# A leaky activation in two ScalarE instructions per tile in place of three

## The chip, the cores and the metric

The kernel runs on one core of a Trainium2 chip. The metric is device time in microseconds (us). The engines are named as in the profile: PE is TensorE (PEld its weight loads), DVE is VectorE, ACT is ScalarE, POOL is GpSimd, SP is SyncE, which here issues DMAs. A change of under 0.3% can't be told from none.

## The reference

Three layers follow each other. The activation that the change touches is in the second.

```
scores = q @ k^T / 8                       # 4 batches x 8 heads, 576 x 576 each, head size 64
keep the 32 largest scores of each row; attn = softmax over them
x  = attn @ v, as 2304 rows of 512
h  = x @ w_in                              # 512 -> 2048
g  = max(h, 0) + alpha * min(h, 0)         # alpha: one number per column of h, drawn from 0 to 0.3
x2 = g @ w_out                             # 2048 -> 512
out = x2, and for the rows with x2 @ w_skip > 0, one of 8 experts (512 -> 1024 -> 512, ReLU)
      is added, weighted with its gate's probability
```

## The kernel before

**Attention.** Work goes in 16 passes of four heads and half the rows of a batch; a pass has nine tiles of 128 rows x 576 scores, in three groups of three tiles. PE makes the scores (L542, L547), ACT stores them (L835). DVE searches the 32nd largest score of each row: four rounds of MAX8 (L1050) with three of MATCH_REPLACE8 (L1063) between them. ACT takes the exponentials (L844) after the first round. DVE masks them and sums them, one SCALAR_TENSOR_TENSOR per tile (L1070, two inputs in SBUF). `invert` (L1079, L1082) makes one over the sums in two tiny DVE operations, put behind the first two MAX8 of the next group. POOL multiplies the tiles by that (L1324), PE transposes them (L560, L561), ACT stores those (L856, L857), and PE multiplies by v (L571).

**The MLP in between.** Two passes make one step of a loop, which runs over eight steps; step 0 has no MLP. From step 1 on, PE also computes the MLP of the half batch that is ready, in an order written out by hand: during the first pass of the step, sixteen tiles of `h` transposed (128 columns of h x 288 rows, twelve fp16 matmuls each, L590, because x and the weights are split into a high and a low fp16 part), during the second pass the product with w_out (L604), then the routing and the rows (L613, L619). There are eight halves: seven in the loop's steps, the eighth after the last attention pass, in the tail.

**The activation before.** For every tile ACT runs three instructions (L882, L883, L886):

```
pos_part = Relu(acc * scale)              # L882, from PSUM
neg_part = Relu(acc * -scale)             # L883, from PSUM, then acc_stored: PE may use the bank again
neg_part = neg_part * (-alpha)            # L886, in SBUF, after a wait for L883; then parts_ready
```

`leak` (L352) follows on POOL, or on DVE for the last half. It waits for parts_ready, adds the two parts (L358, two inputs in SBUF), rounds to fp16 (L360) and subtracts for the low part (L362). POOL does tiles 0 to 4 behind L1324 of the first group of a step, 5 to 11 behind the second, 12 to 15 behind the third (`leak_parts`, L1371). There are four buffers for the parts, and ACT waits for `g_ready` before it writes one again. The instruction order of each engine is fixed; an engine stops at semaphores only.

**Scales.** At the start DVE and ACT take maxima of the weights and of v, POOL spreads them to all partitions over DRAM, and DVE makes powers of two from them (`close_weights` L1097, `scale_weights` L1120). `link_scale` makes an operation of this chain raise a semaphore and DVE wait for it. In step 0 `high_weights` (L927) on ACT multiplies each of eight weight pieces of 128 x 2048 by its scale (L932) and writes the high fp16 part (L936); POOL's `split` (L1334, L1339) writes the low part. The pieces are spread over the groups of step 0, two to a group; the last four are w_out.

Of the kernel before, what the change touches and what calls it, by code (L numbers as in the profile page):

```python
# [24 lines left out]
def topk_attention_prelu_mlp_switch_moe(  # L25
# [17 lines left out]
    ALU = mybir.AluOpType  # L43
    ACT = mybir.ActivationFunctionType
# [53 lines left out]
    with ctx:  # L98
        def sb(name, shape, dt=fp32):
            return ctx.enter_context(nc.sbuf_tensor(name, shape, dt))  # L100
# [69 lines left out]
        neg_scale_g = sb("neg_scale_g", [P, 1])  # L170
        x2_scale = sb("x2_scale", [P, 1])
        neg_alpha = sb("neg_alpha", [P, FT1])
# [111 lines left out]
        parts_ready = sem("parts_ready")  # L284
# [67 lines left out]
        def leak(engine, unit, m, fs):  # L352

            for f in fs:
                n = LEAK_STEPS * (FT1 * m + f)
                pos, neg = pos_part[:, f % NEG, :], neg_part[:, f % NEG, :]
                hold(engine, parts_ready, FT1 * m + f + 1)
# [454 lines left out]
        def _(act):  # L812
# [63 lines left out]
            def mlp_part(m, items, par, part):  # L876
                if par == 0:
                    for f in range(FT1 * part // PARTS, FT1 * (part + 1) // PARTS):
                        n = FT1 * m + f
                        src = begin(items)  # L880
                        act.wait_ge(g_ready, n + 1)
                        nc.scalar.activation(pos_part[:, f % NEG, :], src[:, 0:HALF], ACT.Relu, scale=scale[:, 3:4])  # L882
                        nc.scalar.activation(neg_part[:, f % NEG, :], src[:, 0:HALF], ACT.Relu, scale=neg_scale_g[:, 0:1])\  # L883
                            .then_inc(acc_stored, 1)
                        act.wait_ge(acc_stored, items.base + items.used)
                        nc.scalar.activation(neg_part[:, f % NEG, :], neg_part[:, f % NEG, :], ACT.Copy, scale=neg_alpha[:, f:f + 1])\  # L886
                            .then_inc(parts_ready, 1)
# [39 lines left out]
            def high_weights(i, par, g, half):  # L927
                for n in split_slots.get(GROUPS * (2 * i + par) + g, ())[half:half + 1] if isinstance(i, int) and i < MLP_LAG else ():
                    k = 1 if n < DT else 2
                    act.wait_ge(scale_ready, 1)  # L930
                    act.wait_ge(raw_loaded[n], 16)
                    nc.scalar.activation(raw[:, n, :], raw[:, n, :], ACT.Copy, scale=scale[:, k:k + 1]).then_inc(w_scaled, 1)  # L932
# [101 lines left out]
        def _(dve):  # L1034
# [62 lines left out]
            def close_weights():  # L1097
# [4 lines left out]
                nc.vector.tensor_scalar(neg_alpha[:, :], alpha_sb[:, :], -1.0, None, ALU.mult)  # L1102
# [17 lines left out]
            def scale_weights():  # L1120
                dve.wait_ge(spread_loaded, 16)
                scale_of(1, 3).then_inc(scale_ready, 1)
# [5 lines left out]
                nc.vector.tensor_scalar(neg_scale_g[:, :], scale[:, 3:4], -1.0, None, ALU.mult)  # L1128
# [33 lines left out]
            for m in range(HALVES - MLP_LAG, HALVES):  # L1162
                leak(dve, nc.vector, m, range(FT1))
# [139 lines left out]
        def _(pool):  # L1303
# [68 lines left out]
            with pool.Fori(MLP_LAG, STEPS) as i:  # L1372
                for par in range(2):
                    for g in range(GROUPS):
# [3 lines left out]
                        leak(pool, nc.gpsimd, i - MLP_LAG, leak_parts.get((par, g), ()))  # L1378
# [76 lines left out]
```

## Time and profile before

| what | us |
|---|---|
| median of three runs | 1118.12 |
| lowest and highest | 1116.74, 1120.65 |
| the profiled execution | 1123.2 |
| its span | 1121.4 |
| PE busy | 927.9 (83%) |
| DVE busy | 903.8 (81%) |
| ACT busy | 631.4 (56%) |
| POOL busy | 427.4 (38%) |

The shares are averages over stages of different kinds. Up to about 150 us the weights are made ready beside the first two passes. From 150 to 876 us DVE searches and the MLP runs beside it. From 897 to 950 the last half of the MLP runs alone, and then the experts take the rest of the span. What an engine's busy time is worth has to be read in the stage where it lies.

### The profile page before, as it was taken

The page shows a single profiled execution, that of the slowest core. Times are in us where ns is not written, and L with a number is a line of the kernel's source. Part 1 is how long each engine was busy: PE and PEld are TensorE (multiplying, and loading weights), DVE is VectorE, ACT ScalarE, POOL GpSimd, SP SyncE. Part 2 cuts the span into 40 slices and gives each one's busy share as a digit, 9 for nine tenths or more (in the row PEclk, how much of TensorE's full clock was granted, in tenths as well). Part 3 has the DMA queues.
Part 4 walks back from the last instruction along what each step waited for, and adds up shares of the span by engine and source line. Part 5 has one row for each costly group of instructions (what it writes and reads, how often), then busy time and mean ns, then how long its engine had stood idle before and what let it go on. Part 6 is the DMA issues. An engine that isn't in the chain of part 4 may idle for free.

```text
span 1121.4 us, 22533 instructions
## 1 busy us (share of the span) xinstructions
PE 927.9 (83%) x6271; PEld 616.9 (55%) x6272; DVE 903.8 (81%) x1984; ACT 631.4 (56%) x1324; POOL 427.4 (38%) x598
## 2 busy tenths in 40 slices
PE   5346588898899889888988898899888889498996
PEld 2223256675666657665766575667556567243342
DVE  4999989999999999999999999999999270611110
ACT  3786969647855785587459637954883281010100
POOL 0136738514830682267028513840582100201110
PEclk9956589999999999999999999999999799699999
DMA  7910110013002200310031004001100166626650
GB/s 205 365 37 22 32 34 22 23 41 87 0 21 70 57 0 21 96 32 21 1 97 30 21 8 119 1 21 53 44 2 1 55 226 213 221 90 225 199 165 18
DMA packets 98658, 84.05 MB, mean 75 GB/s; under 512 B 69116, under 2 KB 77308, under 8 KB 98048
## 3 DMA queue, kind: packets, MB, share of 16 engines
q1 hardware_dynamic: 94544, 78.56, 23.0%
q0 software_dynamic: 1488, 3.15, 0.8%
q10 hardware_dynamic: 2528, 1.18, 0.4%
q8 instruction: 43, 0.70, 0.3%
q14 instruction: 55, 0.45, 0.1%
HBM read 72.64 MB, written 11.53 MB: 75 GB/s over the span
## 4 chain that ended last, share of the span: by engine, by line
PE 62%; POOL 12%; issue 11%; ACT 8%; DVE 4%; DMA 2%; POOLq 1%; ACTq 0%; DVEq 0%
PE acc L604 16%; PE acc L571 8%; PE sc L542 7%; PE pt_full L560 6%; PE acc L590 5%; POOL pos_part L358 5%; PE sc L712 3%; PE pt_full L772 3%; POOL arena L360 3%; POOL arena L1324 2%; PE pt_full L780 2%; PE sc L721 2%; PE acc L613 2%; ACT arena L844 1%; PE acc L619 1%
## 5 line engine op out<-in xcount | busy, mean ns | idle before, releaser
L1050 DVE MAX8 best<-arena 128x8 f32<-128x576 f32 x576 | 403.5, 742 | 9.8 <-ACT arena L835 6.6
L1063 DVE MATCH_REPLACE8 arena<-best,arena 128x576 f32<-128x576 f32 x432 | 315.8, 738 | 0.0
L1324 POOL TENSOR_SCALAR arena<-arena,row_inv 128x576 f32<-128x576 f32 x144 | 106.5, 757 | 351.3 <-DVE row_inv L1082 351.3
L590 PE MATMUL acc<-arena 128*128 (+1 forms) x1536 | 202.4, 286 | 28.0 <-ACT neg_part L883 26.1
L604 PE MATMUL acc<-arena 128*128 128x288 f16 x1536 | 202.2, 289 | 2.9 <-issue 2.9
L590 PEld LDWEIGHTS acc<-arena 128*128 128x128 f16 x1536 | 146.4, 98 | 78.8 <-issue 38.9
L604 PEld LDWEIGHTS acc<-arena 128*128 128x128 f16 x1536 | 149.6, 99 | 49.6 <-issue 12.9
L560 PE MATMUL pt_full<-ident,arena 128*128 128x128 f32 x576 | 102.4, 306 | 60.0 <-POOL arena L1324 34.4
L835 ACT ACTIVATE arena<-sc 128x576 f32<-128x576 f32 x144 | 92.1, 642 | 87.1 <-PE sc L542 70.6
L1070 DVE SCALAR_TENSOR_TENSOR arena<-arena,best 128x576 f32<-128x576 f32 x144 | 126.7, 927 | 5.9 <-ACT arena L844 5.9
L560 PEld LDWEIGHTS pt_full<-ident,arena 128*128 128x128 f32 x576 | 73.1, 155 | 90.3 <-POOL arena L1324 42.9
L542 PE MATMUL sc<-kT,qT 64*128 64x288 f32 x512 | 113.0, 478 | 7.0 <-ACT arena L835 5.0
L358 POOL TENSOR_TENSOR pos_part<-pos_part,neg_part 128x288 f32<-128x288 f32 x112 | 96.6, 863 | 48.6 <-ACT neg_part L886 48.6
L571 PE MATMUL acc<-arena,nat 128*64 128x288 f32 (+1 forms) x640 | 92.9, 431 | 20.4 <-ACT arena L857 13.7
L844 ACT ACTIVATE arena<-arena,neg_max 128x576 f32<-128x576 f32 x144 | 101.2, 765 | 1.6
L856 ACT ACTIVATE arena<-pt_full 128x512 f32<-128x512 f32 x128 | 75.5, 590 | 44.3 <-PE pt_rest L561 42.3
L362 POOL TENSOR_TENSOR arena<-pos_part,arena 128x288 f16<-128x288 f32 x112 | 86.7, 774 | 16.7 <-POOL arena L360 1.1
L542 PEld LDWEIGHTS sc<-kT,qT 64*128 64x128 f32 x512 | 63.1, 210 | 39.3 <-issue 20.1
L571 PEld LDWEIGHTS acc<-arena,nat 128*64 128x64 f32 (+1 forms) x640 | 45.0, 141 | 65.0 <-issue 49.8
L882 ACT ACTIVATE pos_part<-acc,scale 128x288 f32<-128x288 f32 x128 | 63.4, 495 | 26.6 <-PE acc L590 25.8
L886 ACT ACTIVATE neg_part<-neg_part,neg_alpha 128x288 f32<-128x288 f32 x128 | 68.5, 535 | 4.2
L883 ACT ACTIVATE neg_part<-acc,neg_scale_g 128x288 f32<-128x288 f32 x128 | 63.1, 493 | 0.0
(172 smaller groups left out, 942.2 us busy)
## 6 DMA issues: line engine op xcount, KB each, us to landing
arena<-in_moe_w_dram SPq DMA_DIRECT2D x64, 512.0 KB, 4.2
nat<-in_v_dram SPq DMA_DIRECT2D x64, 128.0 KB, 2.2
nat<-in_k_dram SPq DMA_DIRECT2D x60, 128.0 KB, 2.8
x_rows<-x2n SPq DMA_DIRECT2D x24, 192.0 KB, 2.4
out_dram<-x2n SPq DMA_DIRECT2D x24, 192.0 KB, 2.6
nat<-in_q_dram SPq DMA_DIRECT2D x64, 64.0 KB, 2.1
arena<-in_moe_w_in_dram SPq DMA_DIRECT2D x4, 1024.0 KB, 7.4
arena<-in_moe_w_out_dram SPq DMA_DIRECT2D x4, 1024.0 KB, 14.5
```

The source lines that it names most:

```text
L358: unit.tensor_tensor(pos, pos, neg, ALU.add).then_inc(leak_ready, 1)
L542: last = nc.tensor.matmul(dst[:, c, 0:HALF], qT[at, h // 2, r * P:(r + 1) * P], kT[at, h // 2, c * HALF:(c + 1) * HALF], start=True, stop= ...
L560: nc.tensor.transpose(pt_full[:, kt, :], src[:, kt * P:(kt + 1) * P], ident[:, :])
L571: last = nc.tensor.matmul(dst[h * D:(h + 1) * D, 0:HALF], v_nat[0:rows, par, 2 * c + h, kt, :], probsT[0:rows, 2 * c + h, kt, :], start=(k ...
L590: last = nc.tensor.matmul(dst[:, 0:HALF], win16[:, a, d, f * P:(f + 1) * P], xT16[:, bass.ds(row + d, 1), b, :].rearrange("p b s -> p (b s)"),
L604: last = nc.tensor.matmul(items.open[:, 0:HALF], wout16[:, a, f // (FT1 // OUT_CHUNKS), f % (FT1 // OUT_CHUNKS) * DM + d * P:f % (FT1 // O ...
L835: nc.scalar.activation(scores[:, t, :].rearrange("p (c s) -> p c s", c=2), sc[(TILES * par + t) % 2][:, :, 0:HALF], ACT.Copy).then_inc(s_s ...
L844: nc.scalar.activation(probs[:, gp, j, :], scores[:, GROUP * g + j, :], ACT.Exp, bias=neg_max[:, gp, j:j + 1], scale=SCALE).then_inc(exp_r ...
L1050: nc.vector.max(best[:, gp, j, r, :], src).then_inc(max_found if r == 0 else dve_step, 1)
L1063: nc.vector.match_replace(left[:, j, :], best[:, gp, j, r, :], src, MASKED).then_inc(dve_step, 1)
L1070: nc.vector.scalar_tensor_tensor(out=probs[:, gp, j, :], in0=tiles[j], scalar=best[:, gp, j, ROUNDS - 1, 7:8], in1=probs[:, gp, j, :], op0 ...
L1324: nc.gpsimd.tensor_scalar(probs[:, gp, j, :], probs[:, gp, j, :], row_inv[:, gp, j:j + 1], 1.0, ALU.mult, ALU.mult)\
```

## The change

With slope = alpha and bend = 1 - alpha, `alpha * h + Relu((1 - alpha) * h)` is h for positive h and alpha * h for negative h. ACT now makes `pos_part` as slope times h (a Copy with a column as scale) and `neg_part` as Relu of bend times h, both from PSUM, and the third instruction goes. For an alpha over 1 a sign is needed, which goes into slope and into the rows of w_out: so w_out's pieces are scaled by a column per 128 rows, in four instructions of 128 x 512 in place of one of 128 x 2048. DVE makes slope, bend and sign at the start. The semaphore parts_ready goes; `leak` waits for acc_stored, which counts tiles of all kinds, so its caller gives the number of the first.

```diff
-                hold(engine, parts_ready, FT1 * m + f + 1)
+                hold(engine, acc_stored, first_item + f + 1)
                 unit.tensor_tensor(pos, pos, neg, ALU.add).then_inc(leak_ready, 1)
...
-                        nc.scalar.activation(pos_part[:, f % NEG, :], src[:, 0:HALF], ACT.Relu, scale=scale[:, 3:4])
-                        nc.scalar.activation(neg_part[:, f % NEG, :], src[:, 0:HALF], ACT.Relu, scale=neg_scale_g[:, 0:1])\
+                        nc.scalar.activation(pos_part[:, f % NEG, :], src[:, 0:HALF], ACT.Copy, scale=slope[:, f:f + 1])
+                        nc.scalar.activation(neg_part[:, f % NEG, :], src[:, 0:HALF], ACT.Relu, scale=bend[:, f:f + 1])\
                             .then_inc(acc_stored, 1)
-                        act.wait_ge(acc_stored, items.base + items.used)
-                        nc.scalar.activation(neg_part[:, f % NEG, :], neg_part[:, f % NEG, :], ACT.Copy, scale=neg_alpha[:, f:f + 1])\
-                            .then_inc(parts_ready, 1)
...
-                    nc.scalar.activation(raw[:, n, :], raw[:, n, :], ACT.Copy, scale=scale[:, k:k + 1]).then_inc(w_scaled, 1)
+                    if n < DT:
+                        last = nc.scalar.activation(raw[:, n, :], raw[:, n, :], ACT.Copy, scale=scale[:, 1:2])
+                    else:
+                        for f in range((n - DT) * FT1 // OUT_CHUNKS, (n - DT + 1) * FT1 // OUT_CHUNKS):
+                            at = slice(f % (FT1 // OUT_CHUNKS) * DM, (f % (FT1 // OUT_CHUNKS) + 1) * DM)
+                            last = nc.scalar.activation(raw[:, n, at], raw[:, n, at], ACT.Copy, scale=sign[:, f:f + 1])
+                    last.then_inc(w_scaled, 1)
...
-                nc.vector.tensor_scalar(neg_alpha[:, :], alpha_sb[:, :], -1.0, None, ALU.mult)
+                link_scale(nc.vector.tensor_scalar(slope[:, :], alpha_sb[:, :], 1.0, None, ALU.min))
+                link_scale(nc.vector.tensor_scalar(sign[:, :], alpha_sb[:, :], 1.0, -2.0, ALU.is_gt, ALU.mult))
+                link_scale(nc.vector.tensor_scalar(sign[:, :], sign[:, :], 1.0, None, ALU.add))
+                link_scale(nc.vector.tensor_tensor(slope[:, :], slope[:, :], sign[:, :], ALU.mult))
+                link_scale(nc.vector.tensor_scalar(bend[:, :], alpha_sb[:, :], -1.0, 1.0, ALU.mult, ALU.add))
...
-                scale_of(1, 3).then_inc(scale_ready, 1)
+                link_scale(scale_of(1, 3))
+                nc.vector.tensor_scalar(sign[:, :], sign[:, :], scale[:, 2:3], None, ALU.mult).then_inc(scale_ready, 1)
...
-                nc.vector.tensor_scalar(neg_scale_g[:, :], scale[:, 3:4], -1.0, None, ALU.mult)
+                nc.vector.tensor_scalar(slope[:, :], slope[:, :], scale[:, 3:4], None, ALU.mult)
+                nc.vector.tensor_scalar(bend[:, :], bend[:, :], scale[:, 3:4], None, ALU.mult)
```

## Rows read from the trace of the kernel before

**Rows 1.** The chain that ended last, its shares of the span by engine.
```profile
PE 62%; POOL 12%; issue 11%; ACT 8%; DVE 4%; DMA 2%; POOLq 1%; ACTq 0%; DVEq 0%
```
**Rows 2.** Windows, DVE alone: window, length, DVE busy (count), clock, DMA share, GB/s.
```profile
255.40:361.20 105.80, 104.41 (x230) 0.98 0.15 40
...
678.70:784.30 105.60, 104.08 (x229) 0.98 0.15 39
```
**Rows 3.** Groups by line: line engine op out<-in xcount | busy us, mean ns | idle before.
```profile
L844 ACT ACTIVATE arena<-arena,neg_max 128x576 f32<-128x576 f32 x144 | 101.2, 765 | 1.6
...
L886 ACT ACTIVATE neg_part<-neg_part,neg_alpha 128x288 f32<-128x288 f32 x128 | 68.5, 535 | 4.2
L882 ACT ACTIVATE pos_part<-acc,scale 128x288 f32<-128x288 f32 x128 | 63.4, 495 | 26.6 <-PE acc L590 25.8 <-POOL arena L362 0.5
...
L871 ACT ACTIVATE x<-acc,scale 128x288 f32<-128x288 f32 x32 | 16.1, 502 | 42.3 <-PE acc L571 42.3
```
**Rows 4.** Timeline of DVE: start us, us, instruction, [idle before it <- releaser].
```profile
184.78 1.16 DVE L1070 SCALAR_TENSOR_TENSOR arena<-arena,best 128x576 f32<-128x576 f32 x1 [0.32 <-ACT arena L844]
...
714.25 1.16 DVE L1070 SCALAR_TENSOR_TENSOR arena<-arena,best 128x576 f32<-128x576 f32 x1 [0.33 <-ACT arena L844]
```
**Rows 5.** Timeline of ACT in the third step of the loop.
```profile
377.45 2.11 ACT L844 ACTIVATE arena<-arena,neg_max 128x576 f32<-128x576 f32 x3
...
380.48 0.49 ACT L883 ACTIVATE neg_part<-acc,neg_scale_g 128x288 f32<-128x288 f32 x1
381.00 0.54 ACT L886 ACTIVATE neg_part<-neg_part,neg_alpha 128x288 f32<-128x288 f32 x1
```
**Rows 6.** Timeline of POOL in the same step.
```profile
381.68 0.81 POOL L358 TENSOR_TENSOR pos_part<-pos_part,neg_part 128x288 f32<-128x288 f32 x1 [1.94 <-ACT neg_part L886]
...
397.29 1.31 POOL L358 TENSOR_TENSOR pos_part<-pos_part,neg_part 128x288 f32<-128x288 f32 x1
...
400.66 0.79 POOL L358 TENSOR_TENSOR pos_part<-pos_part,neg_part 128x288 f32<-128x288 f32 x1
```
**Rows 7.** Two lines of DVE, each by itself: durations in ns, min/median/max.
```profile
L1070 DVE SCALAR_TENSOR_TENSOR arena<-arena,best x144: 790/812/1432, 31.6 to 874.8; 128x576 f32<-128x576 f32 x144
...
L1079 DVE TENSOR_SCALAR row_den<-row_sum x48: 141/150/773, 41.0 to 875.6; 128x3 f32<-128x3 f32 x48
```
**Rows 8.** Timeline of DVE in the same step as rows 5 and 6.
```profile
379.28 1.07 DVE L1070 SCALAR_TENSOR_TENSOR arena<-arena,best 128x576 f32<-128x576 f32 x1
...
396.78 1.16 DVE L1070 SCALAR_TENSOR_TENSOR arena<-arena,best 128x576 f32<-128x576 f32 x1 [0.34 <-ACT arena L844]
...
397.88 1.33 DVE L1070 SCALAR_TENSOR_TENSOR arena<-arena,best 128x576 f32<-128x576 f32 x1
...
399.14 0.96 DVE L1070 SCALAR_TENSOR_TENSOR arena<-arena,best 128x576 f32<-128x576 f32 x1
...
400.71 0.77 DVE L1079 TENSOR_SCALAR row_den<-row_sum 128x3 f32<-128x3 f32 x1
...
419.18 0.59 DVE L1079 TENSOR_SCALAR row_den<-row_sum 128x3 f32<-128x3 f32 x1
```
**Rows 9.** Timeline of DVE before the first step with an MLP.
```profile
48.89 0.16 DVE L1102 TENSOR_SCALAR neg_alpha<-alpha_sb 128x16 f32<-128x16 f32 x1
...
58.66 0.15 DVE L1125 TENSOR_SCALAR power<-spread 128x1 int32<-128x1 int32 x1
58.85 0.15 DVE L1126 TENSOR_SCALAR scale<-power 128x1 int32<-128x1 int32 x1
...
150.46 0.82 DVE L1070 SCALAR_TENSOR_TENSOR arena<-arena,best 128x576 f32<-128x576 f32 x1 [3.37 <-ACT arena L844]
```
**Rows 10.** Timeline of ACT: the scaling of a piece of w_out.
```profile
119.90 1.99 ACT L932 ACTIVATE arena<-arena,scale 128x2048 f32<-128x2048 f32 x1
```
**Rows 11.** Timeline in the tail: the last tile's add, and w_out's first matmuls.
```profile
921.87 0.46 DVE L358 TENSOR_TENSOR pos_part<-pos_part,neg_part 128x288 f32<-128x288 f32 x1 [0.17 <-ACT neg_part L886]
...
923.27 11.90 PE L604 MATMUL acc<-arena 128*128 128x288 f16 x83 [2.93 <-issue]
```

More of the change, by code:

```diff
@@ L169, in topk_attention_prelu_mlp_switch_moe @@
         unscale = sb("unscale", [P, 4])
-        neg_scale_g = sb("neg_scale_g", [P, 1])
         x2_scale = sb("x2_scale", [P, 1])
-        neg_alpha = sb("neg_alpha", [P, FT1])
+        slope = sb("slope", [P, FT1])
+        bend = sb("bend", [P, FT1])
+        sign = sb("sign", [P, FT1])
         x32 = sb("x32", [P, 2, HALF])
@@ L283, in topk_attention_prelu_mlp_switch_moe @@
         x2_written = sem("x2_written")
-        parts_ready = sem("parts_ready")
         leak_ready = sem("leak_ready")
@@ L350, in topk_attention_prelu_mlp_switch_moe, with leak @@
         LEAK_STEPS = 2
-        def leak(engine, unit, m, fs):
+        def leak(engine, unit, m, first_item, fs):
             for f in fs:
@@ L928, in high_weights @@
                 for n in split_slots.get(GROUPS * (2 * i + par) + g, ())[half:half + 1] if isinstance(i, int) and i < MLP_LAG else ():
-                    k = 1 if n < DT else 2
                     act.wait_ge(scale_ready, 1)
                     act.wait_ge(raw_loaded[n], 16)
-                    nc.scalar.activation(raw[:, n, :], raw[:, n, :], ACT.Copy, scale=scale[:, k:k + 1]).then_inc(w_scaled, 1)
+                    if n < DT:
[5 more added lines that the diff above has]
+                    last.then_inc(w_scaled, 1)
                     act.wait_ge(w_scaled, n + 1)
@@ L1162, in _ @@
             for m in range(HALVES - MLP_LAG, HALVES):
-                leak(dve, nc.vector, m, range(FT1))
+                leak(dve, nc.vector, m, TAIL_BASE + PV_ITEMS, range(FT1))
             def link(ins):
@@ L1377, in _ @@
                             low_x(2 * i + par - 1)
-                        leak(pool, nc.gpsimd, i - MLP_LAG, leak_parts.get((par, g), ()))
+                        leak(pool, nc.gpsimd, i - MLP_LAG, LOOP_BASE + (i - MLP_LAG) * FULL_ITEMS + PV_ITEMS + PREP_ITEMS, leak_parts.get((par, g), ()))
             low_x(PASSES_A - 1)
```

## The prediction

> **What bounds the kernel now.** I read the chain of waits first [rows 1]. It gives 62% of the span to PE and 12% to POOL, with ACT at 8%. In a loop where two engines hand work back and forth, such a chain can run along either, so I set the busy times of one loop pass beside it [rows 2]. DVE is busy for 104.4 of 105.8 us in the first and for 104.1 of 105.6 in the last of the five passes from 255 to 784 us. DVE is the bound of the loop: ACT may lose work there without moving the end. So the three ACT instructions of a tile are not priced by their sum. What counts is (a) where DVE waits for ACT, (b) what DVE's own instructions cost, (c) the start, where ACT, POOL and PE form the chain and DVE waits, and (d) the tail, where DVE has little to do.
>
> **The instruction removed.** L886 ran 128 times at 535 ns, 68.5 us of ACT [rows 3]. The Relu L882 becomes a Copy with a column as scale; L871 is such a Copy from PSUM of the same 128x288 and takes 502 ns against 495. That edit costs nothing. Almost all of the 68.5 us lies beside DVE's search and is worth zero.
>
> *(a) DVE's waits for ACT in the loop.* L844 (the exponentials) is queued on ACT behind the tile work. DVE stands 0.32 to 0.34 us for it before one L1070, once in each of six passes (the first and the last of them in [rows 4]). ACT reaches L844 earlier by at least one L886 (0.53 us), so this wait goes: 6 x 0.33 = 2.0 us. After it DVE has only its own work.
>
> *(b) DVE's own instructions.* L1070 takes 0.81 us at its median but up to 1.43, and L1079, a tiny operation, takes 0.15 at its median and up to 0.77 [rows 7]. The slow ones stand beside POOL's leak operations. In one pass: L1070 at 396.78, 397.88 and 399.14 takes 1.16, 1.33 and 0.96, that is 0.35 + 0.52 + 0.15 = 1.0 us more than three medians [rows 8]; POOL's L358, started at 397.29, takes 1.31 instead of its usual 0.80 [rows 6]. L1079 at 400.71 takes 0.77, and POOL's L358 occupies 400.66 to 401.45: L1079 ends when that ends, 0.62 lost. At 419.18 another L1079 takes 0.59 (0.44 lost). The first L1070 at 379.28 loses 0.26. With the three L1070 at the head of the second half (about 1.0 again) that is some 3.4 us in a pass. The pattern is that of taking turns: whichever engine came second stands until the other's instruction is through. What the change does here depends on phase alone, and it shifts POOL's phase.
>
> The shift: the third tile's L883 starts on ACT at 380.48, its L886 at 381.00 and ends at 381.54, and POOL's add starts at 381.68 [rows 5, 6]. After the change POOL waits for the second instruction only (0.53 earlier), and ACT, which had worked without a gap since the tile before, has done one L886 less (0.53 again, and a little of the overlap). POOL's add starts near 380.56, 1.1 us earlier. Now by turns:
> - First window (L1070 from 379.28): the add of tile 1 no longer touches it, gain 0.26. The add at 380.56 now comes in front of the third L1070, which loses 0.52 as the one at 397.88 did, and POOL's subtraction L362, about 2 us after the add with POOL's own stalls in between, then meets L1079 (0.45). Net +0.7.
> - POOL's later tiles run back to back behind this one, so they move earlier by 1.1 less what POOL lost in that window (0.4): 0.7. Second window: DVE starts it 0.7 later but without the 0.33 wait. It now falls so that the first L1070 waits for nothing, the second for 0.15, the third for 0.5: 0.65 in place of 1.0, and L1079 falls at the end of an add (0.05 in place of 0.62). Net -0.33 -0.35 -0.57, and DVE stands 0.6 ahead of before.
> - Third window (L1070 near 415): both engines are 0.6 to 0.7 earlier, same phase, same losses, 0.
>
> Sum of a pass: 0.7 - 0.33 - 0.35 - 0.57 = -0.55, with some -0.6 by the finer addition; over six passes with the wait -3.6 and the seventh without it -0.3: **-3.9 us** for (a) and (b) together. The bounds: if the first window costs 0.7 and nothing is given back, a pass is +0.36 and the loop +2.5; if both hits on L1079 vanish (1.06) with some 0.5 of the L1070s' loss, a pass is -1.1 with half the wait's gain left in it and the loop -8. I take the value that follows the rows at 380.48 and 381.68, since the phase up to there is set by PE, and repeats in every pass.
>
> The Trainium skill (SBUF — State Buffer, section on the two separate sides) says that DVE and GpSimd share one port pair, as an exclusive lock held for a whole instruction, for a DVE operation with two SBUF inputs among others. By that rule the phase decides, as I reckoned above; by a port whose bandwidth is divided, only the overlap would count, and the loop would give about -1.5. L1079, which ends with POOL's add though it moves three numbers, speaks for the lock.
>
> **The edits at the start, all costs.** *DVE.* In place of one unlinked operation (L1102, after which the next starts 0.08 later) come five linked ones. Linked ones of this size follow each other at 0.19 (58.66 to 58.85) [rows 9]: 5 x 0.19 - 0.08 = +0.87. In the scale step one operation gets a link (+0.12), sign times scale comes (+0.07), and two multiplications replace one (+0.07): +0.26. Together +1.1 on DVE at 49 to 59 us. The maxima go to POOL and back by DMA, and DVE's and POOL's next steps all start from these, so the whole chain moves by it.
> *ACT.* Each of the four pieces of w_out is scaled by four instructions of 512 columns instead of one of 2048, which takes 1.99 [rows 10]. From this 2048 and the 288 of L886 (535 ns), both with a column as scale: (1990-535)/1760 = 0.83 ns per column, so 512 columns take 0.72; consecutive ones overlap by 0.1 (L844: three in 2.11 where one takes 0.765 [rows 3, 5]), so 3 x 0.62 + 0.72 = 2.58, +0.6 a piece. Lower bound: no fixed part, +0; upper: no overlap, 2.88, +0.9. Three of the four pieces have ACT on the chain behind them, one has a PE wait of 0.57 that hides it: +1.8. DVE will not hide it: DVE waits at 150.46 for 3.37 us, for ACT's L844 [rows 9], so the chain over ACT, POOL and PE ends last there, and DVE's wait becomes some 5.2. The start costs 1.1 + 1.8 = **+2.9 us**, bounds +1.1 and +3.8.
>
> **The tail.** In the last half's sixteen tiles PE runs from tile to tile without a stop and does not get faster. Only the end moves: DVE's add of the last tile starts at 921.87, just behind L886, and PE starts L604 at 923.27 after standing 2.93 [rows 11]. With L886 gone this is 0.53 earlier: **-0.5 us**. It would be 0 if PE's instruction stream were what stands there, 1.1 if ACT had run one tile behind.
>
> **Sum.** +2.9 - 3.9 - 0.5 = -1.5. The profiled execution took 1123.2 (its span 1121.4 and 1.8 around it) and would take 1121.7. The median of the runs is 1118.1, 5.1 lower with nothing in the trace to say which stage; I carry the difference over: 1116.7.
>
> **Rivals.**
> - *DVE is the bound and POOL's phase brings little* (shared bandwidth, or the hits only move about). For it: the windows are crowded anyway. Against: L1079 at 0.77. Loop -1.5, start +2.9, tail -0.5: +0.9, 1119.0. Chance 0.17.
> - *Relief is larger*: in the first window L1079 misses the subtraction by 0.15 us, which is 0.45 less in each of seven passes: -1.5 - 3.1 = -4.6, 1113.5. A shift in the phase of 0.15 us decides it. Chance 0.22.
> - *Slower*: POOL's earlier adds fall on DVE's L1070 in the first window (+0.7 a pass) and nothing is given back in the second. It decides as soon as the 0.33 and the relief of the second window together fall under 0.3. Loop +2.5, start +2.9, tail -0.5: +4.9, 1123.0. Against it: POOL's whole later stream moves with DVE's. Chance 0.15.
> - *ACT was the bound and gives its time back*, 68.5 us less 2.4: 1052. Against it, DVE busy for 104.4 of 105.8. Chance 0.01. That the edit doesn't shorten ACT's queue at all (Copy at a higher price than Relu) has no row for it and is within the first rival.
>
> **How the numbers follow.** The forecast's case has 0.45, and its own range is 1114 to 1119. A measurement here tells 0.3% (3.35 us) from no change, so faster is under 1114.8 and slower over 1121.5. Faster: all of the larger relief and a sixth of the forecast's case, 0.30. Slower: most of the fourth case and the edges of two others, 0.16. Same: 0.54. The range of eight in ten reaches from the larger relief to just short of the slower case's centre: 1111 to 1122.
>
> **What would show it.** L886 gone, L882 at 0.49 to 0.50. DVE's wait near 150 grown to about 5. POOL's third add 1.1 us earlier against DVE's L1070, the third L1070 of that window at 1.33; no wait of 0.33 before the next window; the sum of L1079's time lower. A pass of about 105.3. The gap before the last half's L604 at 2.4. I am wrong if a pass stays at 105.8 or grows, or if the start costs nothing because DVE's wait there doesn't grow.

## The result, and the profile after

| us | before | after |
|---|---|---|
| median (runs) | 1118.28 (6) | 1126.99 (6) |
| lowest and highest | 1116.64, 1120.65 | 1123.24, 1131.82 |
| the profiled execution, its span | 1123.2, 1121.4 | 1131.8, 1130.0 |
| ACT, DVE, PE busy | 631.4, 903.8, 927.9 | 571.5, 904.8, 939.8 |

The ratio is 1.008, interval [1.0051, 1.0109]: slower by 8.7 us where 1.5 us faster was forecast, and outside the range of 1111 to 1122. The two profiled executions stand 8.6 apart, so they can stand for the runs. ACT did lose 60 us of work. (Ratios leave out runs of more than 1.5% above their kernel's fastest, five of twelve in e11 and three of twelve in e3; these may be part of the effect, so both ratios can understate it.)

The groups by line of the changed kernel (columns as in [rows 3]); ACT's queue is as expected:
```profile
L1072 DVE SCALAR_TENSOR_TENSOR arena<-arena,best 128x576 f32<-128x576 f32 x144 | 130.0, 950 | 16.8 <-ACT arena L844 16.6
...
L882 ACT ACTIVATE pos_part<-acc,slope 128x288 f32<-128x288 f32 x128 | 63.9, 499 | 78.0 <-PE acc L590 61.2
L844 ACT ACTIVATE arena<-arena,neg_max 128x576 f32<-128x576 f32 x144 | 101.2, 765 | 1.6
...
L883 ACT ACTIVATE neg_part<-acc,bend 128x288 f32<-128x288 f32 x128 | 63.2, 494 | 0.0
```
L1072 is the old L1070. DVE stood 16.6 us for L844 ahead of it. Where, the windows of DVE show, one for each of five steps of the loop (a step, two attention passes, is what the prediction calls a pass; columns as in [rows 2]):
```profile
257.30:362.30 105.00, 103.72 (x229) 0.97 0.15 40
362.30:471.30 109.00, 104.70 (x229) 0.94 0.15 38
471.30:578.00 106.70, 104.24 (x230) 0.98 0.15 39
578.00:683.10 105.10, 104.06 (x230) 0.97 0.15 39
683.10:792.20 109.10, 104.78 (x230) 0.94 0.14 37
```
Two steps are shorter than any before (105.6 to 106.0 in windows cut alike), as forecast; three are 1 to 3 us longer, and in them DVE isn't busier to match but stands. DVE's timeline in the second and third of these steps shows for what:
```profile
366.55 0.82 DVE L1072 SCALAR_TENSOR_TENSOR arena<-arena,best 128x576 f32<-128x576 f32 x1 [2.23 <-ACT arena L844]
420.05 0.82 DVE L1072 SCALAR_TENSOR_TENSOR arena<-arena,best 128x576 f32<-128x576 f32 x1 [0.68 <-ACT arena L844]
...
474.80 0.82 DVE L1072 SCALAR_TENSOR_TENSOR arena<-arena,best 128x576 f32<-128x576 f32 x1 [1.42 <-ACT arena L844]
```
ACT, though it has less to do, is late: it waits for PE. The windows of PE (the column after the count is the granted clock), cut where the clock falls and rises, first the kernel before:
```profile
353.10:356.50 3.40, 3.40 (x15) 0.50 0.54 169
```
and the changed one, in the heads of four steps:
```profile
249.40:252.80 3.40, 3.40 (x15) 0.50 0.54 167
355.20:368.90 13.70, 12.52 (x47) 0.50 0.56 151
464.50:471.30 6.80, 6.80 (x24) 0.50 0.72 213
570.30:573.70 3.40, 3.40 (x15) 0.50 0.46 143
```
In every step PE falls to 1.2 GHz (0.50) once, just after the routing product L613, 24 matmuls of nine columns. In the kernel before it is back at 2.4 GHz after 3.4 us, in all six steps. In the changed kernel it stays at 1.2 GHz for 3.4, 13.7, 6.8, 3.4, 13.6 and 13.7 us. What lies there takes longer: forty L571 took 5.52 at 361.24 before, and, with the first 3.5 us of them inside the slow stretch, 7.22 after:
```profile
365.40 7.22 PE L571 MATMUL acc<-arena,nat 128*64 128x288 f32 x40 [1.18 <-ACT arena L857]
```
The sum over DVE's timeline: from the first masking after the start (150.46 before, 153.25 after) to the head of the step at 771.31 (779.51), 620.85 us became 626.26, +5.4; the start +2.8; from there to PE's first L604 of the tail (923.27, 932.29) +0.8; all behind that -0.4. Together 8.6. The +0.8 hides two things: DVE's own last step, with a wait of 2.58 in it, grew by 3.6 (its last masking ends at 875.57 and 887.32), and PE made up 2.7 of it. Of the +5.4, three undisturbed steps gave -0.4 to -0.6 each, and the three disturbed ones took +3.2, +0.5 and +3.1.

### The profile page after: what moved, and what is told of

It is laid out like the page before. It is cut to its first block, busy times and chain, and to the rows that moved or that the text cites. A ratio compares the mean times of both kernels' runs of the same rounds, so it can differ in the third digit from the quotient of the medians.

```text
span 1130.0 us, 22423 instructions
## 1 busy us (share of the span) xinstructions
PE 939.8 (83%) x6271; PEld 621.7 (55%) x6272; DVE 904.8 (80%) x1990; ACT 571.5 (51%) x1208; POOL 432.9 (38%) x598
## 4 chain that ended last, share of the span: by engine, by line
PE 55%; POOL 12%; issue 11%; ACT 10%; DMA 7%; DVE 2%; SPq 1%; POOLq 1%; ACTq 0%; DVEq 0%
PE acc L604 16%; PE acc L571 8%; PE sc L542 7%; DMA arena<-in_moe_w_dram 5%; POOL pos_part L358 5%; PE pt_full L560 5%; PE acc L590 4%; POOL arena L360 3%; PE sc L712 2%; POOL arena L1332 2%; PE pt_full L772 2%; PE acc L613 2%; POOL arena L1347 1%; ACT arena L844 1%; DMA arena<-in_moe_w_out_dram 1%
## 5 line engine op out<-in xcount | busy, mean ns | idle before, releaser
L604 PE MATMUL acc<-arena 128*128 128x288 f16 x1536 | 202.6, 289 | 2.4 <-issue 2.4
L604 PEld LDWEIGHTS acc<-arena 128*128 128x128 f16 x1536 | 149.7, 99 | 49.2 <-issue 12.3
L1072 DVE SCALAR_TENSOR_TENSOR arena<-arena,best 128x576 f32<-128x576 f32 x144 | 130.0, 950 | 16.8 <-ACT arena L844 16.6
L542 PE MATMUL sc<-kT,qT 64*128 64x288 f32 x512 | 118.5, 499 | 6.4 <-ACT arena L835 4.8
L571 PE MATMUL acc<-arena,nat 128*64 128x288 f32 (+1 forms) x640 | 98.4, 451 | 20.8 <-ACT arena L857 13.9
L882 ACT ACTIVATE pos_part<-acc,slope 128x288 f32<-128x288 f32 x128 | 63.9, 499 | 78.0 <-PE acc L590 61.2
L844 ACT ACTIVATE arena<-arena,neg_max 128x576 f32<-128x576 f32 x144 | 101.2, 765 | 1.6
L362 POOL TENSOR_TENSOR arena<-pos_part,arena 128x288 f16<-128x288 f32 x112 | 88.4, 789 | 16.6 <-POOL arena L360 1.1
L571 PEld LDWEIGHTS acc<-arena,nat 128*64 128x64 f32 (+1 forms) x640 | 46.9, 147 | 69.2 <-issue 55.2
L883 ACT ACTIVATE neg_part<-acc,bend 128x288 f32<-128x288 f32 x128 | 63.2, 494 | 0.0
L360 POOL TENSOR_SCALAR arena<-pos_part 128x288 f16<-128x288 f32 x112 | 55.1, 492 | 19.0 <-POOL pos_part L358 19.0
## 6 DMA issues: line engine op xcount, KB each, us to landing
arena<-in_moe_w_out_dram SPq DMA_DIRECT2D x4, 1024.0 KB, 13.6
```

The lines of the kernel that those rows point to most:

```text
L542: last = nc.tensor.matmul(dst[:, c, 0:HALF], qT[at, h // 2, r * P:(r + 1) * P], kT[at, h // 2, c * HALF:(c + 1) * HALF], start=True, stop= ...
L571: last = nc.tensor.matmul(dst[h * D:(h + 1) * D, 0:HALF], v_nat[0:rows, par, 2 * c + h, kt, :], probsT[0:rows, 2 * c + h, kt, :], start=(k ...
L604: last = nc.tensor.matmul(items.open[:, 0:HALF], wout16[:, a, f // (FT1 // OUT_CHUNKS), f % (FT1 // OUT_CHUNKS) * DM + d * P:f % (FT1 // O ...
L844: nc.scalar.activation(probs[:, gp, j, :], scores[:, GROUP * g + j, :], ACT.Exp, bias=neg_max[:, gp, j:j + 1], scale=SCALE).then_inc(exp_r ...
L1072: nc.vector.scalar_tensor_tensor(out=probs[:, gp, j, :], in0=tiles[j], scalar=best[:, gp, j, ROUNDS - 1, 7:8], in1=probs[:, gp, j, :], op0 ...
```

## The experiments

All were timed in five rounds beside the kernel before, whose medians in these sessions were 1118.7 to 1120.6; ratios are to it. "Wait" is DVE's, for L844. After the profile my theory was: **the loop lost because PE stays slow at some heads, and DVE has no slack against the chain over PE and ACT there.** Rivals: the start alone; the DVE/POOL port; the new order on ACT.

**1. exps early.** In steps with an MLP part, the exponentials of the next pass's first group go ahead of that group's stores, in the changed kernel and in the kernel before.
```diff
-                            if j == 0 and not mlp:
+                            if j == 0:
                                 exps(p, par, 0)
...
-                        if mlp:
-                            exps(p, par, 0)
```


> The changed kernel with one move on ACT: in steps with an MLP the exponentials of a pass's first group are issued ahead of the stores of the last group's tiles of the pass before, as in step 0, and no longer behind them. Theory 'clock': what is lost in the loop is that PE stays at 1.2 GHz for up to 13.6 us at the head of some steps, that ACT's exponentials stand in its queue behind stores that wait for this PE, and that DVE waits for them (2.2 to 2.6 us in three steps, 5.1 at the first). Then the waits of DVE for the exponentials at the heads of steps vanish even where PE stays slow: 5.1 at the start, 6.2 to 9 in the loop; about 1127 - 10 = 1117, between 1113 and 1119, faster than the kernel before or level with it. Theory 'port' (DVE's masking is slower by POOL's earlier adds, 130.0 against 126.7 us busy): only the wait at the first step goes, about 1122. Theory 'start only': same, 1122.

> The kernel before with the same move of the exponentials as the first of these runs. It takes away DVE's wait of 3.4 us at 150 us and nothing in its later steps, where DVE didn't wait at the head. All theories: about 1118.3 - 3.4 = 1115. If its steps stay 105.8 long, theory 'clock' expects no long slow stretch to matter; if they come, DVE doesn't wait for them.

Measured 1144.5, 1.021 [1.018, 1.024], and 1160.0, 1.036 [1.033, 1.039]. Both wrong. The waits at the head went, and greater ones came one group later, in both; the kernel before now had one in each step (its timeline of DVE; the masking line is L1069 here):
```profile
391.19 0.82 DVE L1069 SCALAR_TENSOR_TENSOR arena<-arena,best 128x576 f32<-128x576 f32 x1 [5.18 <-ACT arena L844]
```
The three exponentials, 2.1 us of ACT [rows 5], put ahead of the stores delay PE's whole chain. So that chain has no room to spare in the old kernel either; "DVE is the bound" was half of the truth. The steps of e4 took 112.1 to 113.2 us. That is more than the 2.1 that were moved, and PE was at 1.2 GHz for only 3.4 us in those of 112.1 to 112.4; where the rest comes from isn't shown.

**2. The same by one store only**: exps goes just ahead of the last store of scores.

> The changed kernel; in the steps with the second layer, exps of the next pass's first group is issued ahead of the last store of scores of the previous group, and not behind it: it comes about 0.5 us earlier on ScalarE, and only that one store (whose scores VectorE wants last) comes 2.3 us later. If what VectorE lacks at the head of a step after a long stretch of TensorE at 1.2 GHz is only that exps came late, each such wait (1.2 to 2.6 us) gets 0.5 shorter and the kernel gives some 1125 (2 us less). The rival, by the two kernels with exps at the head of the group (1144 and 1160): the chain over ScalarE and TensorE has no room for a shift, the last store is late for the next search, and the time stays at 1127 or grows, with waits for L844 or for the stored scores in the middle of the step.

> The kernel before with the same shift of exps by one store. If room is there, its six waits of 0.33 for L844 shrink or stay and the time is 1117 to 1119. By the rival (the chain is level with VectorE) new waits come in the middle of the step and the time grows past 1122.

Measured 1129.0, 1.0086 [1.0066, 1.0107], and 1121.0, 1.0011 [0.9999, 1.0024]. Nothing gained; in e17 the waits after a slow stretch were 3.3 in place of 2.2 to 2.6, the step still 109.0 to 109.3, and the rival held. e18 fell between its two figures (1119 and 1122) and has no new wait for L844 in the loop, only five of 0.31 to 0.32.

**3. Which part of the change?** e3 scales w_out's pieces by one instruction again, e11 takes the whole start from the kernel before (both leave the sign of an alpha over 1 out, and no alpha is over 0.3), and e12 gives the kernel before the four short instructions only.
```diff
-                        for f in range((n - DT) * FT1 // OUT_CHUNKS, (n - DT + 1) * FT1 // OUT_CHUNKS):
-                            at = slice(f % (FT1 // OUT_CHUNKS) * DM, (f % (FT1 // OUT_CHUNKS) + 1) * DM)
-                            last = nc.scalar.activation(raw[:, n, at], raw[:, n, at], ACT.Copy, scale=sign[:, f:f + 1])
+                    k = 1 if n < DT else 2
+                    nc.scalar.activation(raw[:, n, :], raw[:, n, :], ACT.Copy, scale=scale[:, k:k + 1]).then_inc(w_scaled, 1)
```


> The changed kernel, but each piece of w_out is scaled by one ACT instruction of 2048 columns as before; it leaves out the sign in w_out's rows, which is 1 everywhere for these slopes. By the prediction's step for the start, the wait of DVE at 153 us falls from 5.1 to about 3.3 and the first step with an MLP starts 1.8 us earlier. Theory 'start only': 1125. Theory 'clock, by phase': the first 1.8 us come off too, but the steps also end at other times, so the number of long slow stretches changes in an unforeseen way: between 1116 and 1129.

> The loop part of the change alone: two ACT instructions per tile as in the changed kernel, but at the start DVE makes slope and bend in as many linked steps as before, and each piece of w_out is scaled by one instruction; it leaves out the sign for slopes over 1. By the prediction's steps the start costs 0.1 instead of 2.9 us (DVE's wait near 150 us back to 3.4, the first masking after it at 150.5), and steps without a long stretch are 105.2. Theory 'clock, by phase': long stretches all the same, 1117 to 1130 with a wide spread, median about 1124. Theory 'start only' (the start's 2.8 us and what follows from it are the loss): 1115.

> A start part of the change alone: the kernel before with each piece of w_out scaled by four instructions. By the prediction's step, +1.8 us at the start: DVE's wait near 150 us grows from 3.4 to 5.2. Steps stay 105.8 long. Theory 'clock, by phase': as the slow stage of PE before 150 us carries the start's shift into the step ends, their place can change once, but steps of 105.8 keep it in all steps alike: all short (1120.5) or, if the new place is a bad one, nearly all long (1140). Rival: 1120.5.

Measured 1130.9, 1.0066 [1.0032, 1.0100]; 1132.7, 1.0052 [1.0017, 1.0086]; 1121.0, 1.0018 [0.9989, 1.0047]. e3 and e11 lie above what was expected of them. In e11 the start's cost is gone and the waits are there, at the same places as in the changed kernel:
```profile
148.91 0.82 DVE L1067 SCALAR_TENSOR_TENSOR arena<-arena,best 128x576 f32<-128x576 f32 x1 [3.31 <-ACT arena L844]
...
363.49 0.82 DVE L1067 SCALAR_TENSOR_TENSOR arena<-arena,best 128x576 f32<-128x576 f32 x1 [2.24 <-ACT arena L844]
416.99 0.82 DVE L1067 SCALAR_TENSOR_TENSOR arena<-arena,best 128x576 f32<-128x576 f32 x1 [0.68 <-ACT arena L844]
```
and in e12 only the start's cost:
```profile
152.85 0.82 DVE L1075 SCALAR_TENSOR_TENSOR arena<-arena,best 128x576 f32<-128x576 f32 x1 [4.94 <-ACT arena L844]
```
So the loop part alone brings most of the loss, and the start alone little. The size of the start's cost can't be read from single pairs such as 153.25 against 150.83 (e3) or 152.85 against 150.46: with one and the same start the first masking moves by 2.5 us between profiles (see 7).

**4. Is it the step's length, or ACT's order?** Dead MAX8 instructions on DVE change the length and leave ACT alone: at the end of the step (e2, 480 columns), behind the first pass's third group (e5, and e6 in the kernel before, 512), behind the second pass's second group (e9, e10 in the kernel before, 512; e16, 256).
```diff
+                        if par == 1 and g == 1:
+                            nc.vector.max(spare[:, :], left[:, 0, 0:512])
```


> The changed kernel with one dead instruction on DVE in each step of the loop: a MAX8 over 480 columns into a tile that nobody reads, about 0.56 us, which makes a step without a disturbance as long as before (105.8 instead of 105.2). Theory 'clock, by phase': whether PE's slow stretch at the end of a step is short (3.2 to 3.6 us) or long (6.8, 13.6) depends on when in time the step ends; with steps of 105.8 us all six of the kernel before were short. Then more work makes it faster: long stretches get rare, and the time is about 1118.3 + 2.8 (start) - 0.5 (tail) = 1120.5, 4 to 6 us under the changed kernel. Any theory in which the loop's loss comes from the shorter ACT queue itself, or from the port: 7 x 0.56 = 3.9 us more than the changed kernel, 1131.

> The changed kernel with one dead MAX8 on DVE (512 columns, 0.59 us) in each step of the loop, now inside the step, behind the search of the first pass's third group, where DVE runs without a gap: the dead instruction at the end of the step fell into the idle 1.1 us that DVE has there, and steps without a disturbance stayed at 105.2 to 105.3. Now they are 105.8 to 105.9, as in the kernel before. Theory 'clock, by phase' (short or long stretch at 1.2 GHz depends on when a step ends, and steps of 105.8 keep a good one good): fewer long stretches, faster than the changed kernel in spite of 4 us more work: 1118 to 1123, with a smaller spread. Rival 'the shorter ACT queue makes PE's pattern worse whatever the length of the step': 1127 + 4 = 1131.

> The kernel before with the same dead instruction: steps of 106.4. Work alone: 1119 + 7 x 0.59 = 1123. Theory 'clock, by phase': the good place in time is lost, long stretches come in some steps, 3.3 to 3.7 us each: 1126 to 1132, and a spread as wide as the changed kernel's. Rival: 1123, and every stretch stays at 3.2 to 3.6 us.

> The changed kernel with the dead MAX8 (512 columns, 0.61 us) behind the search of the second pass's second group, where POOL has no leak work that could give the time back by port, and where PE's work for the step's end starts from DVE. The dead instruction of the runs before lay beside POOL's work and was paid back there (L1079 took 0.18 us behind it instead of 0.77), so that steps stayed at 105.2 and 105.8. Now a step without a long stretch is 105.8 to 105.9. Theory 'clock, by phase': stretches at 1.2 GHz stay short where they begin short, median 1118 to 1124 and below the changed kernel's 1127, in spite of 7 x 0.6 us of added work. Rival (the shorter ACT queue itself makes long stretches likely, at any length of the step): 1127 + 4 = 1131, steps of 109.5.

> The kernel before with the same instruction at the same place: steps of 106.4 to 106.5. Work alone gives 1118.7 + 4.3 = 1123, stretches staying at 3.2 to 3.6 us (rival). Theory 'clock, by phase': long stretches in some steps, as in the changed kernel, 1126 to 1134, and a wider spread of the runs than the 7 us of the kernel before.

> The changed kernel with the dead MAX8 at the same place as in the ninth of these runs, of 256 columns (0.33 us): steps of 105.5 to 105.6 without a long stretch, between the changed kernel's 105.2 and the 106.2 of the ninth. Theory 'length of the step': fewer long stretches than the changed kernel or none, 2 to 6 us under it. Rival: 2.3 us over it.

| | median | ratio | undisturbed step | slow stretches at six heads |
|---|---|---|---|---|
| e2 | 1130.1 | 1.0078 [1.0053, 1.0102] | 105.2 | 3.4, 13.6, 13.6, 6.8, 3.4, 13.7 |
| e5 | 1129.5 | 1.0100 [1.0079, 1.0122] | 105.2 | 3.4, 13.7, 13.6, 13.7, 6.9, 3.5 |
| e6 | 1119.0 | 1.0011 [0.9992, 1.0031] | 105.8 | six of 3.4 |
| e9 | 1125.3 | 1.0042 [1.0013, 1.0071] | 106.1 | 3.4, 3.4, 3.5, three with no fall |
| e10 | 1128.3 | 1.0069 [1.0046, 1.0092] | 106.1 | three with no fall, three of 3.4 |
| e16 | 1129.6 | 1.0072 [1.0035, 1.0110] | 105.4 | 3.4, 3.4, 13.6, 13.7, 6.9, 3.5 |

In e2, e5 and e6 the dead work was hidden, in the idle time at the step's boundary or under the port, so the step kept its length and they tested nothing but that. In e9's profile the step is 106.1 to 106.3, and two ScalarE instructions give no long stretch and no wait at a head. The three heads with no fall have none because it moved: falls of 3.4 us lie inside the step, at 517.17 and 622.98, 105.8 apart. With 105.4 to 105.7 (e16) the long stretches come back. By the medians e9 (1125.3) lies just above its theory's range and under the rival's 1131, in spite of 4.3 us of added work: 1.0042 [1.0013, 1.0071] against 1.0103 [1.0071, 1.0135] for the changed kernel in 7. e16 missed: it was to gain 2 to 6 us by fewer long stretches, and has three of them and no gain clear of noise. e10 missed as well: it was to have long stretches and has none, yet it lost 7.7 us where 4.3 us of work were added.

**5. Shorten the old kernel's step.** One tiny DVE operation less in each `invert` (the 1e-9 left out), in the kernel before (e13) and the changed one (e14).
```diff
-                    nc.vector.tensor_scalar_add(row_den[:, gp, :], row_sum[:, gp, :], 1e-9).then_inc(den_ready, 1)
...
-                    nc.vector.reciprocal(row_inv[:, gp, :], row_den[:, gp, :]).then_inc(inv_ready, 1)
+                    nc.vector.reciprocal(row_inv[:, gp, :], row_sum[:, gp, :]).then_inc(inv_ready, 1)
```


> The kernel before, with its three ACT instructions per tile, but without L1079: DVE takes the reciprocal of the row sums directly (it leaves out the 1e-9 in the denominator). That instruction stood for POOL's adds twice in a step, for 0.62 and 0.44 us, and cost 0.06 four more times: steps get about 1.0 us shorter, 104.8. Theory 'length of the step': long stretches at 1.2 GHz now come in this kernel too, DVE waits for L844 at the heads of those steps (2.2 to 2.7 us, never seen in a kernel with three instructions), and the median is 1119 to 1130 in spite of 7 us less work. Rival 'the shorter ACT queue': no long stretches, 1119 - 8 = 1111.

> The changed kernel without L1079, in the same way (the 1e-9 is left out). Steps without a long stretch of about 104.7. Both theories leave long stretches possible: rival 1127 - 5 = 1122 with as many long stretches as the changed kernel; by 'length of the step' their number changes and can't be foretold, 1115 to 1130.

Measured 1119.4, 0.9998 [0.9975, 1.0021], and 1124.0, 1.0041 [1.0013, 1.0068]. e13 missed: the step is 105.7, not 104.8. DVE had 0.9 us less to do in a step, and stood instead (its timeline):
```profile
398.04 1.14 DVE L1070 SCALAR_TENSOR_TENSOR arena<-arena,best 128x576 f32<-128x576 f32 x1 [0.38 <-ACT arena L844]
416.53 0.82 DVE L1070 SCALAR_TENSOR_TENSOR arena<-arena,best 128x576 f32<-128x576 f32 x1 [0.63 <-ACT arena L844]
```
The chain over PE, ACT and POOL, with its fall of 3.4 us in it, is as long as DVE's work in this kernel: about 105.7 a step. e14 missed too: its steps are 105.3 to 106.1, not 104.7. Here the falls, 3.4 long and 105.8 apart, lie in the middle of the step (305.58, 411.40, ...), and DVE waits behind each, 2.0 us for four of five:
```profile
312.04 1.07 DVE L1072 SCALAR_TENSOR_TENSOR arena<-arena,best 128x576 f32<-128x576 f32 x1 [2.01 <-ACT arena L844]
```
So a short stretch, free at a head, costs a wait when it lies elsewhere. This profile is of one of the shorter executions (1117.5, where the median is 1124.0).

**6. Take the fall away.** Fourteen idle fp16 matmuls of 224 columns stand around L613.
```diff
+                fill(8)
...
+                    fill(3 if j else 0)
```


> The changed kernel, with eight idle fp16 matmuls of 224 columns on PE ahead of the routing product of each half (into unused columns of the bank; they lie in the 0.7 us in which PE waits for the last x2T), and three ahead of its second and third group of four matmuls: 0.6 us more on PE in the stage. The routing product is 24 matmuls of 9 columns, and the fall to 1.2 GHz follows on it in every step of both kernels. Theory 'clock': PE falls less often or not at all there, DVE's waits of 2.2 to 2.6 us at the heads of steps go, 1127 - 6 to - 9 = 1118 to 1121. If the fall isn't caused by this stage: 1127 to 1131.

> The kernel before with the same idle matmuls. Its stretches at the ends of steps were short (3.2 to 3.6 us) and DVE hardly waited for them, so little can be won: 1116 to 1120 by theory 'clock'. If the idle matmuls only cost, 7 x 0.6 us on a chain that is level with DVE: 1123.

Measured 1124.7, 1.0049 [1.0025, 1.0074], and 1122.1, 1.0024 [1.0001, 1.0046]. Most falls went, but each kernel has a long stretch at another place (13.7 us at 466.08 and 10.2 at 673.54), with a greater wait: 8.37, and 7.53 in the kernel before. So a kernel with three instructions can meet a long stretch too. Its steps without one are 105.5. DVE in the changed kernel:
```profile
477.42 0.82 DVE L1082 SCALAR_TENSOR_TENSOR arena<-arena,best 128x576 f32<-128x576 f32 x1 [8.37 <-ACT arena L854]
```
By this and e14 a slow stretch seems to cost DVE the more, the further it lies inside the step; no run moved one stretch on its own. The changed kernel's median is 2.3 us lower than without the idle matmuls, but the intervals overlap (1.0025 to 1.0074 and 1.0051 to 1.0109), and it stays behind the kernel before.

**7. The changed kernel once more.**

> The changed kernel itself, unaltered, as the mark for this chip: 1123 to 1132, three to four of six heads of steps with a long stretch.

Measured 1129.9, 1.0103 [1.0071, 1.0135]; stretches 3.4, 13.7, 13.6, 6.8, 3.4, 13.7, nearly the pattern of the first profile. The loop lost the same +5.4 in this profile: from the first masking at 151.08 to the head at 777.30, 626.22 us. The start's +2.8 did not repeat, it is +0.6:
```profile
151.08 0.82 DVE L1072 SCALAR_TENSOR_TENSOR arena<-arena,best 128x576 f32<-128x576 f32 x1 [4.77 <-ACT arena L844]
```
Over all profiles whose start and whose order on ACT are the changed kernel's (after, e2, e5, e7, e9, e14, e15, e16) this masking lies at 150.7 to 153.3, with 151.8 in the middle; over those with the old start (before, e6, e8, e10, e13) at 149.3 to 150.5, with 150.4 in the middle. The start costs some 1.4 us by these middles.

**What a profiled time holds besides.** All that follows from the start of the eighth L613, the routing and the experts, took 165.9 us (e9) to 173.7 (e16) in the twenty profiles, and not by kernel: 172.3 in the kernel before, 167.2 in e6, which has the same steps. The start of that L613 is the better mark of what the change does. The kernel before, the changed kernel and its second profile:
```profile
949.11 2.21 PE L613 MATMUL acc<-wroute,x2T 128*96 128x9 f32 x24 [0.59 <-ACT x2T L890]
958.11 2.21 PE L613 MATMUL acc<-wroute,x2T 128*96 128x9 f32 x24 [0.59 <-ACT x2T L887]
955.78 2.21 PE L613 MATMUL acc<-wroute,x2T 128*96 128x9 f32 x24 [0.59 <-ACT x2T L887]
```
It starts at 949.1 in e6, 949.4 in e14, 952.4 in e9, 954.2 in e10, 955.0 in e11, 955.7 in e16 and 962.6 in e3. The medians, less that of the kernel before in their session, follow roughly: +0.3, +4.3, +4.7, +7.7, +12.1, +9.8 and +11.6. e9's profiled execution took only 1120.0, the best but one of its twelve, because its experts took the least.

**What goes with 3.4 and what with 13.6.** Laid side by side, the sixteen profiles that have L613 in its usual surroundings (without e1, e4, e7, e8) show 84 falls at a head (e14 has its falls elsewhere in the step). What I read in each is the distance from the start of L613 to the fall, as in the first of these two rows of e16's PE and its windows:
```profile
350.34 0.82 PE L614 MATMUL acc<-wroute,x2T 128*96 128x9 f32 x8 [0.68 <-ACT x2T L888]
...
455.84 0.39 PE L614 MATMUL acc<-wroute,x2T 128*96 128x9 f32 x3 [0.68 <-ACT x2T L888]
```
```profile
353.30:356.70 3.40, 3.40 (x14) 0.50 0.57 176
459.10:472.70 13.60, 12.29 (x46) 0.50 0.57 152
```
The distance is 2.96 in the one, and 3.26 in the next. The fall is read to 0.1 us here and in the table; in finer windows 52 stretches of 3.4 us have distances of 1.84 to 2.99, and 32 stretches of 6.8 us and more have 3.09 to 3.58 (those of 6.8 the greatest, 3.50 and above). No case of these lies on the wrong side. It holds for the six heads inside the loop only: at the seventh, where the loop ends and other work follows, e3 has 2.75 and a stretch of 13.7. By step, with the step that follows:

| | distance, fall to fall | step |
|---|---|---|
| before | 2.97, 2.85, 2.80, 2.76, 2.74, 2.72; falls 105.8 apart | 105.6 to 106.1 |
| after | 2.86, 3.45, 3.56, 2.56, 3.24, 3.35; falls 105.8, 109.2, 105.8, 105.8, 109.2 apart | 105.35, 109.07, 106.63, 105.11, 109.08 |
| e13 | 2.14, 2.24, 2.34, 2.48, 2.58, 2.72 | 105.5 to 105.9 |
| e16 | 2.64, 2.96, 3.26, 3.48, 3.54, 2.58 | 105.44, 105.72, 108.72, 109.14, 106.80 |

The falls do not keep the kernel's time. They recur 105.8 us apart though the step is 105.3, so the distance grows by the difference, about 0.5 a step, until it passes 3.0 and PE stays slow. That step is long, the one after 6.8 us throws the distance back by 1.0, and it starts again. The kernel before has a step of 105.8, the same as the distance between falls: its L613 keeps its place, at a good one. Whether that is an accident isn't shown. e6, e12, e13 and e18 have 105.7 to 105.8 on average too, e13 with 0.9 us less for DVE, and so has e14 with its falls inside the step; a chain that holds one fall in each step may settle to the distance between falls, and no run tests it. The Trainium skill (TensorE: Matmul & The Clock Gate, Part 1) says that the clock is set by a watch on the engine's activity that runs free of the program, so that one kernel has a different number of matmuls at the lower clock in different runs. That agrees with falls 105.8 apart at steps of 105.3, and with runs of the changed kernels that lie up to 26 us apart (e11, 1116.4 to 1142.7).

This was read from the profiles once they were there, and is a rule of these cases, not a tested cause. e9 and e16 were built to vary the step's length; no run set the place of L613 by itself. The only three-instruction kernel with a shorter step is e8 (105.5), which has hardly a fall, so that step length and the shorter ACT queue are not separated from that side.

## Why the prediction was wrong

**Right, by its own steps.** *The instruction's durations*: L882 0.50, L883 0.49. *(a)* the six waits of 0.33 [rows 4] are gone. *(b)*, the port's phase: POOL's third add starts 32.58 after the step's head (276.85 less 244.27) in place of 33.74 (275.81 less 242.07), 1.16 earlier, 1.1 forecast. In the first window the third L1072 and the tiny L1081 are hit, in the second L1081 is free:
```profile
277.16 1.34 DVE L1072 SCALAR_TENSOR_TENSOR arena<-arena,best 128x576 f32<-128x576 f32 x1
...
279.11 0.59 DVE L1081 TENSOR_SCALAR row_den<-row_sum 128x3 f32<-128x3 f32 x1
...
293.49 0.87 DVE L1072 SCALAR_TENSOR_TENSOR arena<-arena,best 128x576 f32<-128x576 f32 x1
...
294.29 0.96 DVE L1072 SCALAR_TENSOR_TENSOR arena<-arena,best 128x576 f32<-128x576 f32 x1
...
295.18 1.28 DVE L1072 SCALAR_TENSOR_TENSOR arena<-arena,best 128x576 f32<-128x576 f32 x1
...
297.06 0.14 DVE L1081 TENSOR_SCALAR row_den<-row_sum 128x3 f32<-128x3 f32 x1
```
The third L1072 takes 1.34 as forecast, L1081 0.59 and then 0.14; the second window's three are 0.06, 0.15 and 0.47 over the median, against the 0, 0.15 and 0.5 forecast. The undisturbed step came out at 105.35 and 105.11, against "about 105.3". *The start*, in part by luck: DVE's wait grew to 5.11 and all behind it moved by 2.8, forecast 2.9:
```profile
153.25 0.82 DVE L1072 SCALAR_TENSOR_TENSOR arena<-arena,best 128x576 f32<-128x576 f32 x1 [5.11 <-ACT arena L844]
```
ACT's four instructions took 2.55 a piece, as worked out. But the second profile of the same kernel has +0.6, and the middles over all profiles give +1.4 (experiment 7), half of the forecast. How that divides into ACT's 1.8 and DVE's 1.1 isn't shown. *The tail*: PE stood 2.36 in place of 2.93 [rows 11]:
```profile
932.29 3.92 PE L604 MATMUL acc<-arena 128*128 128x288 f16 x18 [2.36 <-issue]
```

**The step that failed** is the sentence "After it DVE has only its own work", and under it "DVE is the bound of the loop". DVE was busy for 104.4 of 105.8, and I took the chain over PE and ACT as lying somewhere below. It lies at 105.7 in the kernel before (e13) and at the head of a step has no room for 2.1 us (e1, e4). A shorter step was then priced as a gain at every step, while it also moved L613 against PE's falls, and a slow PE for 13.6 us passes straight to DVE: 2.2 to 2.6 us and once more 0.7, a step 3.2 longer than before. I forecast -3.9 for the loop; to the step at 779.5 it gave +5.4. I had not looked at PE's clock inside the steps: the rows of windows showed 0.98 as a mean, and a 3.4 us fall in 105.8 is just that. With each step's fall found, and a chain that is level with DVE, "what if PE were slow for longer" would have been a rival with a price.

**The rivals.** "Slower" named a figure near the result (1123.0), but for another reason: the port gave back in the second window what was forecast, to 0.06 us, so that case was refuted. "POOL's phase brings little" and "larger relief" fell with the measured step. ACT as the bound is excluded by 60 us less of it. Of the sentence "I am wrong if a pass stays at 105.8 or grows", the second part came true in three steps of five.

**Open.** Why the stretch is 13.6 at one distance and 3.4 at another; what the clock did in the executions without a profile (e9's median is 4.7 behind the kernel before and its profile 3.2 at the eighth L613, e10's 7.7 and 5.1, e14's 4.3 and 0.3); whether a three-instruction kernel with a step of 105.3 and its falls in place would lose as much. That long slow stretches pass to DVE and make the steps long is seen in every profile that has them inside the loop; that the step's length brings them on is argued from their places, and from e9 by one profile. No version beat the kernel before.

## What to carry to other kernels

Before pricing a relief, look for a second chain of the same length: take the busiest engine's work away in thought and ask who is late next; in the kernel before it was 0.1 us behind (e13). Look at TensorE's clock in windows of a few us, not in the mean of a stage, and note where the small matmuls are that it falls after. In a loop whose step happens to fit those falls, a step shorter by 0.5% can be a loss; judge it over many executions, and compare profiles at the end of the stage that was changed: here the stage behind it alone differed by up to 7.8 us.

## What the runs showed of the hardware

- An instruction under the port's turn can be free. In e6 a dead MAX8 of 0.68 us stands between the last masking and the tiny operation that had taken 0.77 in the kernel before; that one now takes 0.18, and the step kept its 105.8:
```profile
294.10 0.68 DVE L1158 MAX8 pad<-arena 128x8 f32<-128x512 f32 x1
...
295.37 0.18 DVE L1080 TENSOR_SCALAR row_den<-row_sum 128x3 f32<-128x3 f32 x1
```
- MAX8, with one input in SBUF, was not lengthened beside POOL (0.72 to 0.76 in 576 instructions of the kernel before); the masking with two inputs was (median 0.81, up to 1.43, [rows 7]), and so was a one-input operation on three numbers (0.15 to 0.77) that reads its sums.
- One ACT instruction of 2048 columns took 1.99, four of 512 took 2.55.
- PE's slow stretches at a head inside the loop are 3.4, 6.8 or 13.6 us long in 84 cases (elsewhere also 10.2, as in e8), and the falls at successive heads were 105.8 or 109.2 apart, at steps of 105.1 to 109.2.
